# Gate columns by 32-column weights, three of four groups in slots of the first tile, and an opening written out per engine

## The reference, cut to what matters

```python
# 1. linear attention with decay: 4 batches, 8 heads, 768 steps, 48 dims
for t in range(S):
    cur = u * k_t v_t^T
    y[t] = r_t (state + cur)
    state = w * state + k_t v_t^T
# 2. dense layer over 3072 tokens: 384 -> 2048 -> 384
h = x @ w_in
x2 = (h * sigmoid(h)) @ w_out
# 3. mixture of 8 experts, one expert per token
logits = x2 @ w_gate + modality_bias[modality_id]
e_idx = argmax(logits)
out = gate_w * (relu(x2[mask] @ w1[e]) @ w2[e])
```

## Time and profile before

| | |
|---|---|
| median of 3 runs | 816.91 us (814.11 to 817.08) |
| the profiled execution | 810.66 us, of which the span of instructions is 809.1 |
| slot 0's first matmul in the profile | 42.34 us |
| tile 1's first matmul | 98.81 us |

### The profile page before, as it was taken

The page is one execution under the profiler, slowest core; times in us unless marked ns, Lnnn a source line. Parts: engine busy times, 40 slices in busy tenths (PEclk is TensorE's granted clock), DMA queues, the critical chain, the costliest instruction groups (busy, mean ns, idle before and its releaser), DMA issues. The chain is left out here.

```text
span 809.1 us, 24921 instructions
## 1 busy us (share of the span) xinstructions
PE 755.2 (93%) x9890; PEld 736.4 (91%) x9890; DVE 515.4 (64%) x1367; ACT 432.0 (53%) x1075; POOL 225.9 (28%) x337
## 2 busy tenths in 40 slices
PE   2599999999999999999999999997999999999993
PEld 2599899999999999999998999997899999999992
DVE  7758865685558666766576657424866666566561
ACT  3456463745565545555564546434655655566561
POOL 4421222152214122422224211202324322223321
PEclk9999999999999999999999999997999999999997
DMA  8921222222221222222222210132596766655661
GB/s 319 409 89 38 73 94 73 94 74 93 75 91 43 90 73 93 74 94 73 93 75 61 94 59 12 50 148 71 173 224 212 242 243 210 251 206 197 231 203 70
DMA packets 24159, 104.90 MB, mean 130 GB/s; under 512 B 4411, under 2 KB 9800, under 8 KB 20482
## 3 DMA queue, kind: packets, MB, share of 16 engines
q1 hardware_dynamic: 19362, 93.30, 33.4%
q0 software_dynamic: 4704, 10.29, 4.3%
HBM read 93.86 MB, written 10.11 MB: 129 GB/s over the span
## 5 line engine op out<-in xcount | busy, mean ns | idle before, releaser
L575 ACT ACTIVATE g<-ps_h 128x256 f32<-128x256 f32 x192 | 73.4, 383 | 195.3 <-PE ps_h L893 146.4
L891 PE MATMUL ps_h<-x_hi,wi_hi 128*128 128x256 f32 x576 | 164.6, 286 | 0.0
L892 PE MATMUL ps_h<-x_lo,wi_hi 128*128 128x256 f32 x576 | 162.2, 282 | 0.0
L893 PE MATMUL ps_h<-x_hi,wi_lo 128*128 128x256 f32 x576 | 162.0, 281 | 0.0
L908 PE MATMUL ps_o<-wo_hi,g_hi 128*128 128x392 f32 x384 | 135.4, 353 | 3.6 <-DVE g_lo L746 3.0
L909 PE MATMUL ps_o<-wo_lo,g_hi 128*128 128x392 f32 x384 | 130.5, 340 | 0.0
L910 PE MATMUL ps_o<-wo_hi,g_lo 128*128 128x392 f32 x384 | 130.5, 340 | 0.0
L746 DVE TENSOR_TENSOR g_lo<-g,g_hi 128x256 fp32r<-128x256 f32 x192 | 83.3, 438 | 66.9 <-ACT g_hi L568 65.0
L473 POOL TENSOR_TENSOR store<-store,up_half 128x256 f32<-128x256 f32 x44 | 34.2, 778 | 286.1 <-PE ps_y L878 282.0
L891 PEld LDWEIGHTS ps_h<-x_hi,wi_hi 128*128 128x128 f32 x576 | 109.8, 191 | 1.8 <-issue 1.1
L893 PEld LDWEIGHTS ps_h<-x_hi,wi_lo 128*128 128x128 f32 x576 | 110.1, 191 | 0.0
(11 more groups left out here) (193 smaller groups left out, 1563.3 us busy)
## 6 DMA issues: line engine op xcount, KB each, us to landing
store<-in_w SPq DMA_DIRECT2D x28, 1536.0 KB, 7.1
store<-in_quads SPq DMA_DIRECT2D x48, 704.0 KB, 4.7
x_rows<-rows SPq DMA_DIRECT2D x12, 384.0 KB, 3.2
wi_raw<-in_wi SPq DMA_DIRECT2D x4, 768.0 KB, 10.5
woT_raw<-in_woT SPq DMA_DIRECT2D x4, 768.0 KB, 11.9
wo_raw<-in_wo SPq DMA_DIRECT2D x4, 768.0 KB, 12.5
store<-x_rows,entries POOLq DMA_INDIRECT x26
out_rows<-y,entries_out POOLq DMA_INDIRECT x26, 6.8
```

What stands on the lines that cost most here:

```text
L575: S.activation(g[:, F % 2, :], ps_h[F % 2][:, 0:ETOK], ACT.Silu).then_inc(g_made, 1)
L891: T.matmul(out, hi, x_hi[:, t % 2, c, :], start=(c == 0), stop=False)
L892: T.matmul(out, hi, x_lo[:, t % 2, c, :], start=False, stop=False)
L893: last = T.matmul(out, lo, x_hi[:, t % 2, c, :], start=False, stop=(c == KC - 1))
```

## The change

Ten edits in `front_block`, of three kinds.

**Gate columns.** `gate_columns` becomes `gate_products_of`: the loaded weight is now `w_gate`, padded on the host from 8 to 32 columns, and `woT` is the moving operand, 128 columns at a time; the four blocks go to four groups of 32 columns of the array, so to 32 partitions each of one PSUM tile. ACT copies this tile to SBUF (`copy_gates`), PE transposes it (`turn_gates`), and the split goes on from there. Products in slots 1, 5 and 9, transposes and split two slots later; group 0 lies in the opening.

**The opening.** There are no negative slots any more; each engine has its own written order for units 0 to 3. The fresh states of units 0 to 3 go to `ps_o` and are copied once, in slot 0, by ACT (`first_states`). The values of units 0 to 3 are copied out of `ps_y` by ACT (`copy_front`) and split from the copy. Unit 4's scores move into slot 0, and unit 5's scaling into slots 0 and 1. The masks come before the tables; the tables are written in another order, with `down_made` for what the first transposes need; POOL no longer waits for the tables, and clears 512 instead of 2816 columns of `store`; an early Silu (`warm`) loads ACT's table.

**Transfers.** Quad 3 goes ahead of all weights, and the weights are issued behind the quads' reloads.

```diff
-    GATES_AT = {-1: 0, 1: 1, 5: 2, 9: 3}
+    GATES_AT = {1: 1, 5: 2, 9: 3}
+        gate_product = ps_h[1][:, SIDE:SIDE + P]
+        gate_turn = ps_h[1][:, SIDE + P:SIDE + 2 * P]
+        gate_sums = gate_turn.rearrange("p (f e) -> p f e", e=32)[:, :, 0:E]
...
+            def reload(u):
+                sp.wait_ge(y_done, u + 1)
+                load_quad(u + NQUAD)
...
-            G.memset(z.store[:, SETS:ENDS + 512], 0.0).then_inc(zeros_made, 1)
+            G.memset(z.store[:, ENDS:ENDS + 512], 0.0).then_inc(zeros_made, 1)
...
-            pool.wait_ge(tables_made, 1)
...
+            def copy_gates(i):
+                act.wait_ge(gate_products, i + 1)
+                S.copy(gate_rows[:], gate_product).then_inc(gate_rows_made, 1)
+            def copy_front(u):
+                act.wait_ge(y_done, u + 1)
+                if u >= 2:
+                    act.wait_ge(x_hi_made, u - 1)
+                    act.wait_ge(x_lo_made, u - 1)
+                S.copy(y_front[:, u % 2], ps_y[:, :, 0:C]).then_inc(y_copied, 1)
+            def first_states():
+                act.wait_ge(first_fresh, 4)
+                for c in range(2):
+                    for a in range(2):
+                        last = S.copy(state[c * 64:c * 64 + 64, :, :, a, :],
+                                      ps_o[a * 64:a * 64 + 64, c, :].rearrange("d (p b e) -> d p b e", p=4, b=2))
+                last.then_inc(state_made, 4)
...
-                V.copy_predicated(att[:, u % 2].rearrange("s (a b) t -> s a (b t)", a=2), near_mask[:].rearrange("s (a b) t -> s a (b t)", a=2).bitcast(I16),
-                                  ps_s[:, :, 0:C]).then_inc(att_made, 1)
+                V.copy_predicated(att[:, u % 2].rearrange("s (a b) t -> s a b t", a=2), near_mask[:, None, None, :].to_broadcast([P, 2, 2, T64]).bitcast(I16),
+                                  ps_s[:, :, 0:C].rearrange("s a (b t) -> s a b t", b=2)).then_inc(att_made, 1)
...
-                for f in range(4):
-                    at = SIDE + E * f
-                    for c in range(KC):
-                        last = T.matmul(ps_h[1][:, at:at + E], z.woT[:, i, c, f * P:(f + 1) * P], w_gate[:, c, :], start=(c == 0), stop=(c == KC - 1))
-                last.then_inc(gate_summed, 1)
+                for c in range(KC):
+                    for j in range(4):
+                        last = T.matmul(gate_product[32 * j:32 * j + 32], w_gate[:, c, :], z.woT[:, i, c, j * P:(j + 1) * P],
+                                        start=(c == 0), stop=(c == KC - 1))
+                last.then_inc(gate_products, 1)
+            def turn_gates(i):
+                pe.wait_ge(gate_rows_made, i + 1)
+                T.transpose(gate_turn, gate_rows[:], ident[:]).then_inc(gate_turned, 1)
...
             def fresh_states(u):
-                if u >= 1:
-                    pe.wait_ge(x_lo_made, u)
+                pe.wait_ge(k_end_made, u + 1)
+                if u >= 4:
+                    pe.wait_ge(y_copied if u == 4 else x_lo_made, u)
                     pe.wait_ge(state_made, u)
-                pe.wait_ge(k_end_made, u + 1)
...
+            scores(0)
+            scores(1)
+            fresh_states(0)
+            values(0)
+            gate_products_of(0)
+            scores(2)
+            fresh_states(1)
+            values(1)
+            turn_gates(0)
+            scores(3)
```

More of the change, by code:

```diff
@@ L408, in _ @@
             sp.dma_start(z.modality[:], A["modality"]).then_inc(modality_in, 16)
-            for F in range(FIRST_SLOT, SLOTS + 1):
+            load_turned(1)
+            reload(0)
+            load_up(1)
+            reload(1)
+            load_down(1)
+            load_turned(2)
+            reload(2)
+            load_up(2)
+            load_down(2)
+            reload(3)
+            load_turned(3)
+            load_up(3)
+            load_down(3)
+            for F in range(SLOTS + 1):
                 u = OUTPUT_AT.get(F - 1, QUADS)
                 if u + NQUAD < QUADS:
[L412 to L415, removed]
+                    reload(u)
                 if F == 0:
@@ L550, in x_high @@
                         act.wait_ge(x_hi_part, u + 1)
[L551 removed]
+                    last = S.copy(x_hi[q:q + n, t % 2, c, :].rearrange("d (c n) -> d c n", c=2), y[first:first + n])
                     if n == 64:
@@ L587, in _ @@
             S.copy(end_tab[:].rearrange("s p a d -> s (p a d)"), ps_y[:, 0, :]).then_inc(end_made, 1)
[L588 to L593, removed]
+            set_diagonal(0)
+            halves()
+            set_diagonal(1)
+            wi_high(0)
+            copy_front(0)
+            x_high(0)
+            set_diagonal(2)
+            copy_gates(0)
+            wi_high(1)
+            copy_front(1)
+            x_high(1)
+            set_diagonal(3)
+            gate_high(0)
+            wo_high(0)
+            copy_front(2)
+            x_high(2)
+            wi_high(2)
+            copy_front(3)
+            x_high(3)
+            wi_high(3)
+            for F in range(SLOTS):
                 t, f = divmod(F, FCH)
@@ L756, in bias_of_tokens, with scale @@
                 link(V.tensor_tensor(z.bias_of[:], z.bias_of[:], part[:], ALU.add))
+            make_masks()
             make_tables()
-            make_masks()
-            dve.wait_ge(zeros_made, 1)
-            for F in range(FIRST_SLOT, SLOTS):
+            def scale(u):
+                scale_a(u)
+                scale_b(u)
+            scale(0)
+            sum_bonus(0)
+            scale(1)
+            sum_bonus(1)
+            near(0)
+            scale(2)
+            sum_bonus(2)
+            near(1)
+            wi_low(0)
+            x_low(0)
+            scale(3)
+            sum_bonus(3)
+            near(2)
+            wi_low(1)
+            x_low(1)
+            near(3)
+            gate_low(0)
+            wo_low(0)
+            x_low(2)
+            wi_low(2)
+            scale(4)
+            sum_bonus(4)
+            x_low(3)
+            wi_low(3)
+            for F in range(SLOTS):
                 t, f = divmod(F, FCH)
```

256 lines of the change are left out of this document (150 added, 106 removed).

## The result

The changed kernel took 812.57 us (median of 20 runs, 809.86 to 816.17), the kernel before 816.23 on the same chip (20 runs, 812.07 to 825.12). The ratio is 0.9948 [0.9933, 0.9964]: 4.2 us gained by it (3.7 by the medians), where 11.6 were forecast. The profiled execution took 811.17 us, of which the span is 809.6; that of before had a span of 809.1, but its execution was faster than every other run of its kernel on that chip. The two chip conditions differ by some 7 us for both kernels, so ratios are compared here. Tile 0 doesn't depend on it: in e8, from the other condition, its four windows take 13.21, 13.53, 12.37 and 17.34 us, as in the first profile of the changed kernel.

A forecast was written before the change was run, and what follows sets the result against it. PE, busy for 93% of the span, was taken as the bound, with DVE next; 7.5 + 1.1 + 3.0 = 11.6 us off 816.91 gave 805.3, stated as 805.5 us, range 800 to 813 for 8 in 10.

The forecast's parts named there:

- E: Tile 0, slots 4 to 11: cheaper gate blocks save about 1.5 us per four-slot window, limited by DVE; 3.0 us gained.
- everything behind tile 0 is unchanged work and should only shift: After tile 0: the rest of the span stays as long as before, 710 us.
- A: Opening: masks ahead of re-ordered tables and less clearing by POOL bring first scores from 13.80 to about 10.0 us.
- C: Price of a gate block: 1.5 us at the low clock, 0.8 at the high, plus 0.3 and 0.15 for the transpose.
- its 1.8 us: Gate blocks: possible cost of array mode switches, 0.6 per group less old block ends; left out of the sum, kept in the range.
- Rivals 1 and 2: Gate product runs serially, 814.5 us, chance 0.09; slot 0 stays tied to the weight loads' end, 812.5 us, chance 0.12.
- Rival 4: Tile 0: PE's clock stays low, about 1.9 us more per slot, 820 us with eight slots; chance 0.05.
- Rival 3: Opening: breaks vanish or clock rises early, slot 0 at 32.5, slots 0 to 3 in 12, total 801 us; chance 0.12.
- B: Opening, units 0 to 3: slot 0 begins at 34.8 instead of 42.34 us, 7.5 us gained.
- instruction breaks: Opening: PE runs out of instructions in scores 2 and at the end of scores 3, as before for 2.31 and 2.14 us.
- D: Tile 0, slots 0 to 3: 15.1 us becomes 14.0, including 0.5 for ACT's first_states; 1.1 us gained.

The follow-up runs named there:

- e8: Changed kernel with two 48-byte pads, so x_hi and the g buffers lie 1344 and 1280 bytes from their old places; 801.09 us, ratio 0.9882.
- e7: Kernel before, with only POOL's scaling of units 6 to 9 put behind DVE's near; 807.73 us, ratio 0.9991.
- e1: Changed kernel with POOL's scaling of units 6 to 9 put behind DVE's near of the same unit; 800.83 us, ratio 0.9881.
- e3: Changed kernel with every old SBUF buffer at its old address, by pads and new buffers last; 801.70 us, ratio 0.9891.
- e4: Changed kernel again, unchanged, on a second chip; 803.20 us, ratio 0.9928 to the kernel before.
- e11: Changed kernel a third time, unchanged, under the slower chip condition; 810.81 us, ratio 0.9946 to the kernel before.
- e10: e6 with POOL's routing constants moved one unit later; 798.49 us, ratio 0.9853 to the kernel before.
- e6: Changed kernel with both mends, POOL's later scaling (e1) and the old SBUF addresses (e3); 798.19 us, ratio 0.9869 to the kernel before.

## Why the prediction was wrong

**The failed step is E**, "4 to 11 in about 23 us with DVE hardly idle". Its PE side was right: 23.04 us of work in two windows, forecast 2 x 11.3 = 22.6. Its DVE side took the 11.1 to 11.7 us per four slots from the earlier trace rows as a fixed amount that could be laid beside less PE work. It was measured at a period in which POOL's work fell only partly on operations that suffer from it (e7 puts that part at 0.7 and 0.6 us per window). In the shorter period more of DVE's SBUF subtractions met POOL, and its work rose to 13.11 and 11.84 us, of windows of 13.59 and 12.35. The step gave 0 instead of 3.0, and cost 1.9 in the last window, about which the prediction said that it "stays". With POOL moved (e1) slots 4 to 11 take 24.04 us, 1.9 of the 3.0, and the last window has 15.52; the 1.02 us of idle time that e1 leaves in slot 5 no run removes.

**Second, "everything behind tile 0 is unchanged work and should only shift."** It was unchanged work at other addresses, for 0.3 us per odd tile and 2 us in all (e3, e8). No row of the kernel before could have shown it. Behind tile 0 the first profiles have 717.5 instead of 710.3 us; the rest of that is for the most part ACT's stand in tile 10 and the longer time behind the last Silu, which come with the chip condition, and so no step of the prediction.

**A, C, right.** First scores at 10.55 against about 10.0; products 1.51 and 0.86 us against 1.5 and 0.8; the transpose 0.47 against 0.3. From the product's start to the next matmul are 1.43 us. PE's work in slots 4 to 11 fell by 2.88 where the sum has 3.3 (twice 1.65), so about 0.2 us per group is left for changes of array mode, less than half of the 0.45 by which the prediction reckoned its 1.8 us. Rivals 1 and 2 fell with these rows and slot 0 at 35.64. Rival 4 fell as a whole: in the first profile the up step behind the product of slot 5 has its matmuls 0.12 us apart. A piece of it is real, though: in e3, e4 and e11 the clock fell again for 3.4 us behind the wait at that product and cost PE 1.5 us. Rival 3 was right in that one break nearly vanished, but slots 0 to 3 took 13.21 us, not 12.

**B, right but for 0.8.** Slot 0 came 6.7 us earlier, forecast 7.5. Both instruction breaks were where they were put, the second 0.46 long instead of about 2. That gave back 1.5 us. Against it stands DVE, which has no idle time from 29.72 until `x_low(3)` ends at 35.58: beside POOL's multiplications `wi_low` took 1.30 instead of 0.55, unit 4's scaling 0.80 and 1.94 instead of 0.43 and 1.02, and `x_low(3)` 1.68 instead of 1.29, 2.4 us in all, and 2.4 less 1.5 is about the 0.8. `x_low` can be stretched here because the change gave it a copy in SBUF to read instead of PSUM. The routing constants aren't to blame: `x_low(2)` beside them kept 1.29, and when e10 took them away slot 0 didn't move, while the multiplications stayed. No run moved those, so this account is argued from rows and not shown.

**D, right in sign, too small.** 1.93 instead of 1.1: the estimated 0.5 for ACT's `first_states` wasn't paid, PE being busy in all 13.21 us. The other 0.3 lies within the sizes of the terms (1.43 for the product, and a transpose at the upper clock).

**The sum.** Forecast were 7.5 + 1.1 + 3.0 = 11.6. By the rows of the first profiles slot 0 gave 6.7, slots 0 to 3 1.9, slots 4 to 11 nothing, the last window took 1.9 back, and the addresses took 2.0: 4.7 us, and the three ratios say 4.2, 4.4 and 5.8. With both mends the same change gives 10.6 us (e6) and 11.9 (e10) by their ratios. That this is about the 11.6 is partly luck: slot 0 and slots 4 to 11 still give less than forecast and slots 0 to 3 more, and a ratio is sure to 2 us only.

## What to carry to other kernels

When a change takes work off PE, sum the next engine's work anew for the new period, with each of its operations at the length it has beside what then runs on POOL; a mean over windows in which it had slack is no bound. Schedule POOL's work beside DVE operations that read PSUM: in e1 `x_low` (from PSUM) kept its 1.30 us beside POOL. Before tile times of two profiles are compared, look at the granted clock of their windows: here a fall of 3.4 us hid in them. And when buffers are added or resized, keep those that PE reads at their place within 64 bytes, or put the new ones last.

## What the runs showed that was not expected

- Addresses: 41.9 instead of 41.6 us for an odd tile with matmul operands shifted by 1392 and 1376 B, 41.5 at 1344 and 1280 B, 41.75 with a shift of 16 B in the kernel before.
- DVE and POOL: subtractions from SBUF at 0.82 to 1.10 instead of 0.42 to 0.55 us, and POOL's own multiplications at 0.85 and 0.92; in e1, behind `near`, they took 0.74 and 0.60:

```profile
61.29 0.74 POOL L507 TENSOR_TENSOR store<-store,up_half 128x256 f32<-128x256 f32 x1 [8.80 <-DVE att L792]
61.99 0.60 POOL L512 TENSOR_TENSOR store<-store,end_tab 128x192 f32<-128x192 f32 x1
```

- Parts of the array: 24 fp32 records of 128 columns with 32-column weights take 1.43 us at the low clock and 0.79 at the high one until the next matmul starts, against 5.1 and 2.6 for 128x8 records with full 128x128 weights.
- The granted clock fell to 0.50 for 3.4 us in three of six profiles in which PE had waited 2.03 to 2.11 us at one place, and the tile ended 1.1 us sooner in these three.
- ACT stood for 5.8 us in two of three profiles of one kernel, at one and the same instruction, where a weight transfer lands in 9.0 to 9.1 instead of 7.2 us, and not in the third or in any other run. What it waited for is open.
